# A linear-attention and two-MLP kernel: y of the odd head pairs goes to a second PSUM bank with its rows exchanged, and the order of the start and of the last products is rewritten

## The reference, cut to what matters

```python
# r, k, v, w: (4, 8, 768, 48); u: (8, 48)
for t in range(S):                                   # gated linear attention, state 48 x 48 per head
    cur = einsum('bhd,bhe->bhde', u[None] * k[t], v[t])
    y[t] = einsum('bhd,bhde->bhe', r[t], state + cur)
    state = w[t][..., None] * state + einsum('bhd,bhe->bhde', k[t], v[t])
x = y as (3072, 384)
h = x @ w_in;  g = h * clip(h + 3, 0, 6) / 6;  x = g @ w_out          # w_in (384, 2048)
out = ((x @ w1) * (x @ w2)) @ w3 @ w_out2                             # w1, w2 (384, 1024), w3 (1024, 1024)
```

## Time and profile before

| | |
|---|---|
| three runs, median | 935.88 us (934.26 to 936.74) |
| the profiled execution, time | 930.96 us |
| its span | 929.2 us |
| TensorE, VectorE, ScalarE, GpSimd busy | 905.5, 554.9, 314.3, 268.9 us (97%, 60%, 34%, 29% of the span) |
| instructions | 22908 |

### The profile page before, as it was taken

How to read it: one execution, slowest core, us unless ns; L and a number is a source line. 1 busy time by engine, 2 the same in 40 slices (tenths; PEclk the granted TensorE clock), 3 DMA queues, 4 the chain that set the end, 5 groups by cost and what they waited for, 6 DMA issues and landing times.

```text
span 929.2 us, 22908 instructions
## 1 busy us (share of the span) xinstructions
PE 905.5 (97%) x9992; PEld 815.5 (88%) x9992; DVE 554.9 (60%) x746; ACT 314.3 (34%) x508; POOL 268.9 (29%) x209
## 2 busy tenths in 40 slices
PE   8898989999999999999999999999999999999998
PEld 4566889999999999989999999998888888888887
DVE  5888996878687888787888753552222221322221
ACT  0324433343433343333334343543122222222212
POOL 0665736363536363636363600000000000000000
PEclk9989999999999999999999999999999999999999
DMA  9996524343434444334344101531020202000000
GB/s 299 339 287 210 151 71 144 95 147 106 133 95 126 122 125 117 117 105 128 109 123 118 40 21 35 167 123 52 1 68 1 68 1 68 1 35 1 5 30 34
DMA packets 62482, 93.29 MB, mean 100 GB/s; under 512 B 7927, under 2 KB 48462, under 8 KB 62382
## 3 DMA queue, kind: packets, MB, share of 16 engines
q1 hardware_dynamic: 59390, 88.16, 31.5%
q10 hardware_dynamic: 2992, 3.67, 1.3%
HBM read 76.07 MB, written 11.01 MB: 94 GB/s over the span
## 4 chain that ended last, share of the span: by engine, by line
PE 78%; DVE 12%; POOL 2%; DMA 2%; issue 2%; SPq 1%; ACT 1%; DVEq 0%; POOLq 0%
PE ps_acc L1061 11%; PE ps_acc L1062 9%; PE ps_acc L1063 9%; PE ps_h L1063 9%; PE ps_h L1062 9%; PE ps_h L1061 9%; PE ps_lv L1062 4%; PE ps_lv L1063 4%; PE ps_lv L1061 4%; PE ps_lv L1097 3%; DVE k_sb L791 2%; DVE r_sb L791 2%; PE ps_acc L1133 2%; PE ps_acc L1141 2%; DVE A_own L882 2%
## 5 line engine op out<-in xcount | busy, mean ns | idle before, releaser
L527 POOL TENSOR_TENSOR tok_a<-tok_a 128x384 f32<-128x384 f32 x126 | 169.2, 1369 | 208.7 <-DMA tok_a<-in_k 208.7
L570 ACT ACTIVATE g_hi<-gated 128x512 fp32r<-128x512 f32 x144 | 91.0, 632 | 248.6 <-PE ps_acc L1063 124.5
L1061 PE MATMUL ps_acc<-g_hi,w_out_hi 128*128 128x256 f32 x576 | 170.2, 296 | 0.0
L1061 PE MATMUL ps_h<-x_hi,w_in_hi 128*128 128x256 f32 x576 | 162.8, 283 | 3.1 <-ACT w_out L570 3.1
L1062 PE MATMUL ps_h<-x_hi,w_in_lo 128*128 128x256 f32 x576 | 162.7, 283 | 0.0
L1063 PE MATMUL ps_h<-x_lo,w_in_hi 128*128 128x256 f32 x576 | 162.6, 282 | 0.0
L1062 PE MATMUL ps_acc<-g_hi,w_out_lo 128*128 128x256 f32 x576 | 162.0, 281 | 0.0
L1063 PE MATMUL ps_acc<-g_lo,w_out_hi 128*128 128x256 f32 x576 | 161.4, 280 | 0.0
L1043 DVE TENSOR_TENSOR gated<-gated,ps_lv 128x512 f32<-128x512 f32 x48 | 33.0, 688 | 188.5 <-PE ps_lv L1063 188.5
L1061 PEld LDWEIGHTS ps_acc<-g_hi,w_out_hi 128*128 128x128 f32 x576 | 108.3, 188 | 5.2 <-issue 2.0
L968 DVE TENSOR_TENSOR g_lo<-gated,g_hi 128x512 fp32r<-128x512 f32 x96 | 76.8, 800 | 59.9 <-ACT g_hi L570 59.9
(11 more groups left out here) (94 smaller groups left out, 1607.8 us busy)
## 6 DMA issues: line engine op xcount, KB each, us to landing
tok_a<-in_r SPq DMA_DIRECT2D x21, 768.0 KB, 4.2
tok_a<-in_w SPq DMA_DIRECT2D x21, 384.0 KB, 4.8
v_sb<-in_v SPq DMA_DIRECT2D x12, 384.0 KB, 3.8
x_scratch<-x_out SPq DMA_DIRECT2D x12, 384.0 KB, 4.3
x_in<-x_scratch SPq DMA_DIRECT2D x6, 768.0 KB, 6.1
tok_a<-in_k SPq DMA_DIRECT2D x22, 192.0 KB, 5.0
out<-x_out SPq DMA_DIRECT2D x5, 768.0 KB, 4.0
x_sb<-y_sb SPq DMA_DIRECT2D x138, 24.0 KB, 2.3
```

The source lines that it names most:

```text
L527: return nc.gpsimd.tensor_tensor(dst, x, y, ALU.mult)
L570: return nc.scalar.activation(dst, src, ACT.Copy, **scale)
L1061: nc.tensor.matmul(psum, hi, moving_hi, start=start, stop=False)
```

## The change

Seven edits come together.

1. y of the odd pairs (a = 1, 3) goes to the second bank of `ps_lv` instead of `ps_att`, and head h of an odd pair takes the other 64 rows. `y_copy` becomes two copies; the DMAs of x read the rows by `y_row`. The new states of both chunks move to the first bank, `update` waits for both chunks' new states, `read` waits for `turn_out`, and step 0 of the next group waits for `y_out`. Group 1 uses other banks for its levels.
2. `sum_bands(2p + 3)` moves from READ_A to READ_B, one slot later, behind `update`.
3. The first scalings (stages 0 and 1 of group 0) become `first_scalings`: the four operations on totals and k come before the wait for r.
4. Order on VectorE in the head: `update(0)`, `keep(1)`, `update(1)`, `scale(1, 1)` come ahead of `sum_bands(1)` and `start(1)`; `gate(0)` comes ahead of `sum_bands(4)`. W_HEAD is 9.
5. On ScalarE each `store_w34` from the fourth on stands earlier, and `split_weight(8)` comes after `clip(0)`, `split_weight(9)` inside the first slot.
6. On TensorE `attention(0, READ_B)` comes after `attention(1, 0)` and one half of `form_w34`; two `keep_busy` matmuls are left out.
7. The last products of the second MLP: `product(46)`, `product(47)`, then the three sums `project2(45)`, `(46)`, `(47)`.

```diff
-W_HEAD = 10
+W_HEAD = 9
+        def y_row(a, h):
+            return (a + h) % 2 * HB
+        def y_bank(a):
+            return ps_lv[:, 1, :] if a % 2 else ps_att
+        def y_cols(a):
+            return slice(a // 2 * C, (a // 2 + 1) * C)
+        def new_state(p, c):
+            return banks_of(p, READ_A)[:, 0, c * PAIRS * D:(c + 1) * PAIRS * D]
...
-                copy(flat(y_sb[g % 2]), ps_att[0:HP, :]).then_inc(y_out, 1)
+                for odd in range(2):
+                    last = copy(y_sb[g % 2][:].rearrange("d (a two) t -> d two a t", two=2)[:, odd],
+                                y_bank(odd)[0:HP, 0:2 * C].rearrange("d (a t) -> d a t", t=C))
+                last.then_inc(y_out, 1)
...
+            def first_scalings():
+                k_g, r_g, w_g = flat(k_sb[0]), flat(r_sb[0]), flat(w_sb).rearrange(
+                    "d (m two) -> d m two", two=2)
+                t_g = totals_of(0).rearrange("d (m two) -> d m two", two=2)
+                wide = [HP, PAIRS * GT // 4, 2]
+                dve.wait_ge(d_loaded[0], GROUP_D)
+                times(totals_of(0), w_g[:, :, 0], w_g[:, :, 1]).then_inc(head_totals, 1)
+                times(halves(k_g, 1)[:, :, 0, 0], halves(k_g, 1)[:, :, 0, 0], w_g[:, :, 1]
+                      ).then_inc(head_totals, 1)
+                dve.wait_ge(head_totals, 2)
+                times(totals_of(1), t_g[:, :, 0], t_g[:, :, 1])
+                times(halves(k_g, 2)[:, :, 0, :], halves(k_g, 2)[:, :, 0, :],
+                      t_g[:, :, 1].unsqueeze(2).to_broadcast(wide))
+                dve.wait_ge(r_loaded[0], GROUP_R)
...
-                dve.wait_ge(state_products, updates(g))
+                dve.wait_ge(state_products, updates(2 * p + 1))
...
                     if p + 1 < GROUPS:
                         scale(p + 1, 1)
-                    sum_bands(2 * p + 3)
                 if step == READ_B:
                     update(2 * p + 1)
+                    sum_bands(2 * p + 3)
...
             start(0)
             scale(1, 0)
-            sum_bands(1)
-            start(1)
             update(0)
             keep(1)
             update(1)
             scale(1, 1)
-            split_weight(0)
+            sum_bands(1)
+            start(1)
             scale(1, 2)
             merge(1, 0)
+            split_weight(0)
...
             split_weight(5)
+            split_weight(6)
+            split_weight(7)
+            gate(0)
+            split_weight(8)
             sum_bands(4)
-            for q in range(6, 10):
-                split_weight(q)
-
-            gate(0)
...
+                    pe.wait_ge(y_out, 2 * p)
                     pe.wait_ge(merged[(p - 1) % 2], level(p - 1, LEVELS - 1))
...
+                if c == 0 and p > 0:
+                    pe.wait_ge(k_turns_out, updates(2 * p + 1))
...
-                            ps_att[h * HB:(h + 1) * HB, a * C:(a + 1) * C],
+                            y_bank(a)[y_row(a, h):y_row(a, h) + HB, y_cols(a)],
...
-                                ps_att[rows, a * C:(a + 1) * C], state[g % 2][rows, a, :],
+                                y_bank(a)[y_row(a, h):y_row(a, h) + D, y_cols(a)], state[g % 2][rows, a, :],
...
             form_w34(3, 0)
-            attention(0, READ_B)
             attention(1, 0)
             form_w34(3, 1)
+            attention(0, READ_B)
...
-            for n in range(2, OUT_TILES * NF2):
+            for n in range(2, OUT_TILES * NF2 - 1):
                 product(n)
-                project2(n - 1)
-            project2(OUT_TILES * NF2 - 1)
+                if n < OUT_TILES * NF2 - 2:
+                    project2(n - 1)
+
+            product(OUT_TILES * NF2 - 1)
+            for n in (3, 2, 1):
+                project2(OUT_TILES * NF2 - n)
```

More of the change, by code:

```diff
@@ L294, in banks_of @@
         def banks_of(p, step):
-            if p == 1 and step in (1, 3):
+            if p == 1 and step in (0, 2):
                 return ps_acc[:, 0:2, :]
@@ L388, in move_x @@
                 for head in range(H // 2 if g < 2 else H):
-                    row, at_row = head * D, head % 2 * HB
+                    row, at_row = head * D, y_row(head // 2, head % 2)
                     while row < (head + 1) * D:
@@ L707, in _ @@
             split_weight(0)
+            store_w34(3)
             y_copy(1)
@@ L711, in _ @@
             split_weight(2)
-            store_w34(3)
+            store_w34(4)
             split_weight(3)
             split_weight(4)
-            store_w34(4)
             merge(1, 2)
+            store_w34(5)
             split_x(0)
             split_x(1)
-            store_w34(5)
             split_weight(5)
             merge(1, 3)
+            store_w34(6)
             split_weight(6)
-            store_w34(6)
             split_weight(7)
-            split_weight(8)
-            split_weight(9)
             store_w34(7)
@@ L813, in scale @@
                       ).then_inc(scaled[p % 2], 1)
+            def first_scalings():
[12 more added lines that the diff above has]
+                dve.wait_ge(r_loaded[0], GROUP_R)
+                times(halves(r_g, 1)[:, :, 1, 0], halves(r_g, 1)[:, :, 1, 0], w_g[:, :, 0]
+                      ).then_inc(scaled[0], 1)
+                dve.wait_ge(scaled[0], stage(0, 0))
+                times(halves(r_g, 2)[:, :, 1, :], halves(r_g, 2)[:, :, 1, :],
+                      t_g[:, :, 0].unsqueeze(2).to_broadcast(wide)).then_inc(scaled[0], 1)
             def head_products_by_token(g):
@@ L901, in update @@
                 p, c = divmod(g, 2)
-                new = banks_of(p, READ_A)[0:HP, c, 0:PAIRS * D].rearrange("d (a e) -> d a e", a=PAIRS)
-                dve.wait_ge(state_products, updates(g))
+                new = new_state(p, c)[0:HP, :].rearrange("d (a e) -> d a e", a=PAIRS)
+                dve.wait_ge(state_products, updates(2 * p + 1))
                 if not takes_state(g):
@@ L973, in _ @@
             nc.vector.memset(y_sb[0][:], 0.0).then_inc(y_zeroed, 1)
-            scale(0, 0)
-            scale(0, 1)
+            first_scalings()
             scale(0, 2)
@@ L1073, in level_products @@
                         pe.wait_ge(merged[0], level(0, step - 3 if step == 3 else step - 2))
+                elif p == 1 and step == 0:
+                    pe.wait_ge(state_new, updates(1))
                 elif p == 1 and step == 1:
-                    pe.wait_ge(state_new, updates(1))
+                    pe.wait_ge(y_out, 2)
                 elif p == 1 and step in (2, 3):
@@ L1079, in level_products @@
                     pe.wait_ge(merged[p % 2], level(p, step - 1))
-                elif p == 1:
-                    pe.wait_ge(merged[0], level(0, 1))
                 else:
+                    pe.wait_ge(y_out, 2 * p)
                     pe.wait_ge(merged[(p - 1) % 2], level(p - 1, LEVELS - 1))
@@ L1133, in read @@
                         last = nc.tensor.matmul(
-                            ps_att[h * HB:(h + 1) * HB, a * C:(a + 1) * C],
+                            y_bank(a)[y_row(a, h):y_row(a, h) + HB, y_cols(a)],
                             v_sb[:, first:first + HB], A_own[:, h, c, a, :],
-                            start=(a == 0), stop=not takes_state(g), skip_group_check=True)
+                            start=(a < 2), stop=not takes_state(g), skip_group_check=True)
                 if takes_state(g):
@@ L1155, in new_states @@
                                 last = nc.tensor.matmul(
-                                    banks_of(p, READ_A)[h * HB:(h + 1) * HB, c, a * D:(a + 1) * D],
+                                    new_state(p, c)[h * HB:(h + 1) * HB, a * D:(a + 1) * D],
                                     k_turned[:, c, at_col:at_col + HB], v_sb[:, first:first + D],
```

7 lines of the change are left out of this document (4 added, 3 removed).

## The result

The changed kernel takes 918.22 us in the median (916.89 to 923.84, 4 runs), the kernel before 935.07 us beside it (931.56 to 936.74). The ratio is 0.9841 with a 95% interval of 0.9815 to 0.9867: 14.9 us faster (12.4 to 17.3). The forecast was 919 in a range of 911 to 929. In a later comparison the same kernel had 0.9832 (0.9795 to 0.9868).

The account below looks back on a forecast made before the run. TensorE, busy 97% of the span, was taken as the bound, with VectorE bounding part of the head. Head 7.0, state reads 7.5, stall 2.4 and tail 0.3 sum to 17.2 us: 935.9 - 17.2 = 918.7, about 919; range 911 to 929.

Parts of the forecast that it names:

- The state reads: TensorE's state reads use all four array quarters at once: 0.44 us less each, 17 reads, 7.5 us.
- Rival B: State reads do not overlap further, as products between share output rows and switch bank: 926 us, chance 0.10.
- F: Each bank change costs a 0.11 us change-over in both reads and state reads gain nothing: 944 us, chance 0.04.
- The A reads: TensorE's A reads still use two array halves, only in another order: priced at 0, at worst 0.33 us per chunk.
- D: Only the A read suffers from its new order, 6.6 us in all: 926 us, chance 0.07.
- C: Strict program order: no gain in 17 state reads, 0.33 us more in 20 A reads: 933 us, chance 0.08.
- The stall: TensorE's wait before step 2 of the levels shrinks 0.3 us for 8 groups: 2.4 us, bounds 0 and 6.3.
- The head: VectorE's idle pieces from 41 us on go, so TensorE is 7.0 us earlier at 127.7; bounds 3 and 11.
- my signs of being wrong: A read 1.35 us, state read 1.01, TensorE waiting for ScalarE's y, or VectorE idle for GpSimd at the fourth band sum.
- E: Head gains 2 us instead of 7, as VectorE next meets a DMA or ScalarE: 924 us, chance 0.09.
- A: Everything goes as forecast: 919 us, own range 912 to 926, chance 0.62.
- The tail: End of the second MLP: TensorE's wait for the last g_lo and weight loads behind it go, 0.3 us gained.

Follow-up runs that it names:

- grouped: Changed kernel with A products ordered half by half and state products quarter by quarter, same addresses; 934.23 us, ratio 0.9985 to the kernel before.
- before: The kernel before, without any of the seven edits; median 935.07 us, its profiled execution 930.96 us.
- y_two_banks: Kernel before with only y of the odd pairs in the second bank with rows exchanged; 926.18 us, ratio 0.9919.
- sum_later: Kernel before with only the odd chunk's band sum moved from READ_A to READ_B; 932.64 us, ratio 0.9988.
- tail_alone: Kernel before with only the last three sums of the second MLP put behind the last two products; 935.03 us, ratio 1.0013.
- after: The changed kernel with all seven edits; median 918.22 us, ratio 0.9841 to the kernel before, its profiled execution 919.46 us.
- after_again: The changed kernel, unchanged, measured once more in a later comparison; 919.8 us, ratio 0.9832 to the kernel before.
- head_alone: Kernel before with only the head's new orders on VectorE, ScalarE and TensorE, W_HEAD 9 and two keep_busy fewer; 929.27 us, ratio 0.9952.
- sum_back: Changed kernel with the odd chunk's band sum back in READ_A; 921.66 us, ratio 0.9858 to the kernel before.
- band4_later: Changed kernel with the fourth band sum moved from ahead of the slots into the first slot; 919.58 us, ratio 0.9825 to the kernel before.
- weights_first: Changed kernel with four weight loads ahead of the tok_b load in SyncE's queue; 920.4 us, ratio 0.9845 to the kernel before.
- filled: Changed kernel with three unused matmuls before TURN of group 1 and before step 2 of group 2; 917.72 us, ratio 0.9815 to the kernel before.

## Why the prediction was right, point by point

**The state reads** (7.5 in the sum): right in mechanism and size. 17 reads gave 7.2 us, 0.42 each, and the part alone 7.6. Rival B (no further overlap) and F (a change-over at each bank) are refuted by 0.58 us with four starts within 0.02.

**The A reads** (0): 1.02 to 1.03 us, so D does not hold for low, high, high, low. `grouped` shows that it was no empty worry: an order with longer runs on one half costs 0.49 us per read. C, strict order, is refuted by the state read. Of the Trainium skill's rule that matmuls start in program order ("TensorE: Matmul & The Clock Gate", "Part 3: Packing small matmuls — row/col tiling"), the strict reading does not fit the 0.58 us; that order counts at all is what 1.51 us shows.

**The stall** (2.4, bounds 0 and 6.3): 2.9 in the profiled pair. Over all executions with both edits the stalls are 3.1 to 4.9, with one or none of them 5.4 to 7.9; `grouped`, which has both but long A reads, has 6.8. The working held in its detail: in five of eight groups GpSimd begins together with or behind x_lo, and this needs the late sum and the shorter reads.

**The head** (7.0): the term that was mis-sized. The part alone measured 4.5 us; at the place that I named the profiled pair has 2.7, under my lower bound of 3. Over four executions of the old order (`before`, `y_two_banks`, `sum_later`, `tail_alone`) step 2 of group 2 comes at 127.4 to 131.5 us, over six of the new order (`after`, `after_again`, `head_alone`, `sum_back`, `band4_later`, `weights_first`) at 123.1 to 126.6, the means some 4.5 us apart. The step that failed is "Together 6.14 + 0.95 = 7.1": it takes VectorE's idle pieces as the gain, as if nothing came in their place. It also left out two pieces, 0.54 us at 47.53 and 0.70 at 91.18. The reason that I gave for the largest piece, "because `sum_bands(4)` now has `gate(0)` and three weight splits ahead of it, about 4 us", held in `after_again`, `head_alone` and `weights_first`, where VectorE waits no more, and not in the profiled changed kernel (1.87 us, one of my signs of being wrong) nor in `sum_back` (4.75 us). These executions reach step 2 of group 2 at 126.55, 123.08, 124.92, 125.03 and 123.36 us, so the piece was no measure of the gain. In its place came other waits (1.29 us for ScalarE, which issues the moves of x before it splits the weight, and 0.41 + 1.28 us for ScalarE's clip and TensorE's new states, behind the long wait of TURN), slower work beside GpSimd, and in the changed kernel a `tok_b` load that left 3 us later in SyncE's queue, which I had priced at 0 by leaving it out. So E, "VectorE, freed of two waits, meets a DMA or ScalarE at the next one", describes the head better than A, though its gain of 2 us is too small. What sets the head's length from one execution to the next stays open.

That the stall of `hidden(1)` goes on to `hidden(2)` and TURN was right, its size varies: 0.9 and 5.4 us in the profiled changed kernel, 3.4 and 1.5 in `after_again`, for 1 and 3 to 4 forecast. I gave no price to what a long wait does to the clock: 1.5 us in the `project` behind the 3.29 us wait. `filled` shows that the cost goes when the wait is filled.

**The tail** (0.3): the last wait is gone, the stretch from the last READ_B on is 0.4 us shorter in the profiled pair, and alone no gain can be measured.

**The sum.** 17.2 us were forecast from the median, 14.9 (12.4 to 17.3) measured. That 919 came within 1 us of the median is in part luck: the two medians of that comparison differ by 16.9 us, the ratio gives 14.9, and 2.5 to 4 us too much for the head stood against a stall 0.5 us too small. My own range for A was also added up wrongly: with 3 to 11 and 0 to 6.3 it is 911 to 925, not 912 to 926.

## What to carry to other kernels

Give neighbouring small products different quarters of the array: the second bank alone gained nothing in the read, with the exchanged rows it went from 1.01 to 0.58 us. When a hand-written order is changed, price the queue behind the moved instruction on every engine, the DMA queue first, and expect a removed pause to come back at the next meeting of the engines, or as slower work of VectorE beside GpSimd. Where TensorE must wait some us in such a stretch, matmuls whose result is not used kept its clock here, and it is the work behind the wait that gained (1.5 us in one `project`; the ratio of the whole moved within its interval).

## What the runs showed of the hardware that was not expected

After 3.29 us without work TensorE's next `project` ran at a granted clock of 0.55 and took 3.76 us instead of 2.24; with unused matmuls in the wait the clock was 1.00. A wait of 2.65 us at the same place in `tail_alone` was followed by 0.56, one of 2.83 us in `y_two_banks` by 1.00. Three weight splits of VectorE took 5.1 us beside GpSimd in `after_again`; in `sum_back` they took 2.69 us and it was GpSimd's products that took longer. The same products took 1.02 or 1.51 us by their order alone when they used two halves of the array, but 0.58 or 0.60 when they used four quarters; why the quarters bear long runs and the halves do not is left open.
